# Low tail products of two up-projection steps set among attention scores, two attention chunks begun a step later

## The reference

```python
# 1: gated linear attention (mLSTM) per head, written as a recurrence over t
C = f_stab * C + i_stab * outer(v_t, k_t);  n = f_stab * n + i_stab * k_t
y_t = sigmoid(o_t) * (C @ q_t) / max(|n . q_t|, 1)
# 2: a dense layer pair, 320 -> 2048 -> 320
h = x @ w_in;  x = (h - tanh(h)) @ w_out
# 3: four experts, 320 -> 1024 -> 320, mixed by given probabilities
out += p[:, e] * (relu(x @ w1[e]) @ w2[e])
```

## Time and profile before

| | us |
|---|---|
| median of 3 runs | 585.32 |
| lowest, highest | 584.59, 585.38 |
| the profiled execution | 584.94 |
| its span, first to last instruction | 583.1 |
| TensorE matmuls busy | 579.0 |
| VectorE, ScalarE, GpSimd busy | 222.2, 200.9, 128.5 |

### The profile page before, as it was taken

How to read it: one execution, slowest core, us unless ns; L and a number is a source line. 1 busy time by engine, 2 the same in 40 slices (tenths; PEclk the granted TensorE clock), 3 DMA queues, 4 the chain that set the end, 5 groups by cost and what they waited for, 6 DMA issues and landing times.

```text
span 583.1 us, 8971 instructions
## 1 busy us (share of the span) xinstructions
PE 579.0 (99%) x3658; PEld 528.1 (91%) x3658; DVE 222.2 (38%) x449; ACT 200.9 (34%) x399; POOL 128.5 (22%) x102
## 2 busy tenths in 40 slices
PE   9999999999999999999999999999999999999997
PEld 8899999999998888899999999999999999999997
DVE  6657656565555333413131313131323232222222
ACT  5785655565444555511123211123211111111111
POOL 4888333332200444400004300014300000000000
PEclk9999999999999999999999999999999999999999
DMA  7987735664210222300002300001000000001011
GB/s 277 349 289 254 273 106 169 168 168 97 52 40 0 75 96 98 127 5 1 0 1 99 100 1 0 1 1 49 2 1 1 1 0 1 1 0 46 1 45 46
DMA packets 39054, 44.33 MB, mean 76 GB/s; under 512 B 21190, under 2 KB 31686, under 8 KB 39014
## 3 DMA queue, kind: packets, MB, share of 16 engines
q1 hardware_dynamic: 38912, 43.71, 23.3%
q10 hardware_dynamic: 102, 0.05, 0.0%
HBM read 39.02 MB, written 4.73 MB: 75 GB/s over the span
## 4 chain that ended last, share of the span: by engine, by line
PE 99%; DVE 0%; issue 0%; ACT 0%; DVEq 0%
PE bank L1321 11%; PE bank L1320 11%; PE bank L1322 11%; PE bank L1376 10%; PE bank L1375 10%; PE bank L1374 10%; PE bank L1323 6%; PE bank L1324 6%; PE bank L1346 5%; PE bank L1347 4%; PE bank L1348 4%; PE bank L1118 2%; PE bank L1354 2%; PE bank L1355 2%; PE bank L1161 1%; PE bank L1132 1%
## 5 line engine op out<-in xcount | busy, mean ns | idle before, releaser
L1094 DVE SCALAR_TENSOR_TENSOR g_lo<-bank,g_hi 128x512 fp32r<-128x512 f32 x96 | 66.4, 692 | 253.4 <-ACT g_hi L815 253.4
L815 ACT ACTIVATE g_hi<-bank 128x512 fp32r<-128x512 f32 x96 | 57.5, 599 | 269.8 <-PE bank L1324 269.7
L1376 PE MATMUL bank<-w_all,g_lo 128*128 128x320 f32 x384 | 118.7, 309 | 0.0
L1375 PE MATMUL bank<-w_all,g_hi 128*128 128x320 f32 x384 | 118.5, 309 | 0.0
L1321 PE MATMUL bank<-x_lo,w_all 128*128 128x512 f32 (+2 forms) x318 | 118.2, 372 | 0.0
L1374 PE MATMUL bank<-w_all,g_hi 128*128 128x320 f32 x384 | 118.2, 308 | 0.0
L1320 PE MATMUL bank<-x_hi,w_all 128*128 128x512 f32 (+2 forms) x318 | 117.9, 371 | 0.0
L1322 PE MATMUL bank<-x_hi,w_all 128*128 128x512 f32 (+2 forms) x318 | 117.0, 368 | 0.0
L598 POOL TENSOR_TENSOR w_all<-w_raw,w_all 128x1408 fp32r<-128x1408 f32 x16 | 51.7, 3233 | 192.3 <-ACT w_all L687 192.3
L1374 PEld LDWEIGHTS bank<-w_all,g_hi 128*128 128x128 f32 x384 | 72.1, 188 | 3.7
L1375 PEld LDWEIGHTS bank<-w_all,g_hi 128*128 128x128 f32 x384 | 72.1, 188 | 3.7
(11 more groups left out here) (161 smaller groups left out, 646.0 us busy)
## 6 DMA issues: line engine op xcount, KB each, us to landing
w_raw<-in_w SPq DMA_DIRECT2D x24, 704.0 KB, 4.3
zb<-z SPq DMA_DIRECT2D x10, 512.0 KB, 5.3
feat<-in_feat SPq DMA_DIRECT2D x10, 512.0 KB, 4.1
tok<-in_tok SPq DMA_DIRECT2D x10, 484.0 KB, 4.8
spare<-xg SPq DMA_DIRECT2D x8, 256.0 KB, 2.8
out<-arena SPq DMA_DIRECT2D x12, 160.0 KB, 1.9
fb<-f SPq DMA_DIRECT2D x16, 80.0 KB
xg<-feat SPq DMA_DIRECT2D x16, 80.0 KB
```

What stands on the lines that cost most here:

```text
L815: A(g_hi[:, b, 0:N], h_ps[b][:, 0:N], ACT.Relu).then_inc(ghi_ready, 1)
L1094: V.scalar_tensor_tensor(g_lo[:, b, 0:N], h_ps[b][:, 0:N], 0.0, g_hi[:, b, 0:N].bitcast(F32), ALU.max, ALU.subtract).then_inc(g_ready, 1)
L1375: mm(out, g_hi[:, b, t], low_w, start=False, stop=False)
L1376: last = mm(out, g_lo[:, b, t], high_w, start=False, stop=stop)
```

## The change

Each of chunks 6 to 11 names a step `m = START[n] + 1`, the step of its scores: with the new `START`, 19, 23, 27, 32, 36 and 39. In `up(m)` and in `up(m+1)` the matmul L1324 is left out. In its place the scores hold two pairs of half-size matmuls, `halves`: each has 64 rows and half of the 384 columns, one in the lower and one in the upper 64 partitions, and one writes to the bank of step m, the other to that of step m+1. The first pair comes after two of the eight score matmuls and begins the bank of step m+1 there; the second comes after six and ends that of step m, so that `h_ready` of step m is now given there. That the upper 64 rows can be used asks for the high tail there: for the second half of the columns of a group `x_low` now writes the low tail in the lower 64 partitions. The middle chunks 3 and 6 are written in two pieces for it. Chunks 9 and 10 begin a step later (31 and 35), so that steps m and m+1 always belong to one group.

```diff
-START = {2: 3, 3: 7, 4: 10, 5: 14, 6: 18, 7: 22, 8: 26, 9: 30, 10: 34, 11: 38}
+START = {2: 3, 3: 7, 4: 10, 5: 14, 6: 18, 7: 22, 8: 26, 9: 31, 10: 35, 11: 38}
...
+def tail_parts(n):
+    if n in (3, 6):
+        return (True, slice(0, CH // 2)), (False, slice(CH // 2, CH))
+    return (n not in (4, 7), slice(0, CH)),
...
+        in_halves = [START[n] + 1 for n in range(6, STEPS)]
...
-                V.scalar_tensor_tensor(x_hi[64:P, 2, c], turn[64:P, 2, :], 0.5, x_hi[64:P, 2, c].bitcast(F32),
-                                       ALU.mult, ALU.subtract).then_inc(xlo_done, 1)
+                for above, t in tail_parts(n):
+                    half, ct = slice(64, P) if above else slice(0, TAIL), slice(n * CH + t.start, n * CH + t.stop)
+                    last = V.scalar_tensor_tensor(x_hi[half, 2, ct], turn[half, 2, t], 0.5,
+                                                  x_hi[half, 2, ct].bitcast(F32), ALU.mult, ALU.subtract)
+                last.then_inc(xlo_done, 1)
...
+            def halves(m, here, there):
+                N = width(m)
+                c, half = span(m).start, N // 2
+                mm(h_ps[here % 2][:, 0:half], up_part(here, 1, 2)[0:TAIL, :], x_hi[0:TAIL, 2, c:c + half],
+                   start=False, stop=False)
+                return mm(h_ps[there % 2][:, half:N], up_part(there, 1, 2)[64:P, :], x_hi[64:P, 2, c + half:c + N],
+                          start=there != m, stop=there == m)
...
                 r = n % RING
+                m = START[n] + 1 if n >= BATCH else -1
...
+                    if j == 0 and m in in_halves:
+                        pe.wait_ge(g_ready, m)
+                        halves(m, m, m + 1).then_inc(halves_begun, 1)
+                    if j == 2 and m in in_halves:
+                        pe.wait_ge(halves_begun, in_halves.index(m) + 1)
+                        halves(m, m + 1, m).then_inc(h_ready, 1)
                 last.then_inc(s_ready, 1)
...
+                begun = m - 1 in in_halves
                 for k in range(2 if m else 0):
-                    mm(h, up_part(m, 0, k), x_hi[:, k, c], start=k == 0, stop=False)
+                    mm(h, up_part(m, 0, k), x_hi[:, k, c], start=k == 0 and not begun, stop=False)
...
-                mm(h, up_part(m, 0, 2), x_hi[:, 2, c], start=False, stop=False)
-                mm(h, up_part(m, 1, 2), x_hi[:, 2, c], start=False, stop=True).then_inc(h_ready, 1)
+                last = mm(h, up_part(m, 0, 2), x_hi[:, 2, c], start=False, stop=begun)
+                if begun:
+                    last.then_inc(h_ready, 1)
+                elif m not in in_halves:
+                    mm(h, up_part(m, 1, 2), x_hi[:, 2, c], start=False, stop=True).then_inc(h_ready, 1)
```

More of the change, by code:

```diff
@@ L272, in mlstm_mlp_experts @@
         part_lo = sem("part_lo")
+        halves_begun = sem("halves_begun")
         xhi_done = sem("xhi_done")
```

## The result

| | before | after |
|---|---|---|
| median, us | 585.21 | 589.13 |
| lowest, highest (6 executions each) | 584.49, 585.38 | 586.89, 591.13 |
| the profiled execution, its span | 584.94, 583.1 | 586.89, 585.0 |
| TensorE matmuls busy, by the page | 579.0 | 577.9 |

The ratio after to before is 1.0071, interval 1.0053 to 1.0088: 0.7% slower, where 586.7 us (+0.3%) was forecast with a range up to 588.0. The direction is right, and the profiled execution, 586.89, lies on the forecast. But it is the fastest of the six; the median lies 2.4 us above the forecast and outside its range. So two questions are open: whether the sum held in the execution that was profiled, and what the other executions have that it has not.

A forecast was written before the change was run, and what follows sets the result against it. TensorE's matmuls, busy 99% of the span, were taken as the bound. Terms -0.81 + 0.15 - 0.12 + 0.03 + 0.34 + 2.2 = +1.8 on 584.94 gave 586.7 us; range for 8 in 10: 584.9 to 588.0.

The forecast's parts named there:

- What bounds the kernel: Whole kernel: TensorE's matmuls are busy 579.0 us, 99% of the span, so only removed matmuls or new standstills change the time.
- The pairs: Among the scores, six times: two pairs at 0.107 us each replace two matmuls at 0.174; net -0.81 us.
- that rival (0.02): Around the scores: 64 and 40 rows are two tiling modes and TensorE drains between them, +3.6 us, 590.3; chance 0.02.
- the one with dear pairs: Among the scores: pairs don't run side by side or wait for their weights, 0.174 or more each, 587.7 us; chance 0.06.
- The self-wait: In the scores: the second pair waits for the first, with 0.1 us to spare; nothing, at most 0.1 each.
- `h_ready(m)` late: After the scores: h_ready comes some 0.9 us later, delaying tanh, subtraction and g_lo, but TensorE has other work; nothing.
- `down(32)`: Between down(31) and down(32): the sums of chunk 9, moved there, cover the wait for the evacuation; -0.12 us.
- (a) `state_ready`: Step 39, before the scores of chunk 11: they wait for finish_state(10), now at the end of step 38's VectorE work; +0.34 us.
- (b) the denominators: DMA queue, steps 39 to 43: chunk 11's denominators are read at 161.98, land at 164.3 and delay down(43); +2.2 us.
- the wait at step 31: Scores at step 31: the first pair waits for g_ready, late because of step 30's VectorE work; +0.15 us.
- two plain steps: Steps 30 and 34 now end with x_low and no scores behind; weights come slightly late, +0.03 us net.
- the DMA chain is slower: DMA queue before down(43): other transfers lengthen a leg by 1 us and the stall equally, 587.7 us; chance 0.15.

The follow-up runs named there:

- the repeat: The changed kernel measured once more, unchanged, against the kernel before: 589.63 us, ratio 1.0092.

## Why the prediction was right, and where it failed

- **What bounds the kernel** held: each us of standstill on TensorE came out as a us of time.
- **The pairs** were sized nearly rightly: 0.11 us each against 0.107, and 0.174 for what they replace. Net -0.6 against -0.81 over six places. The Trainium skill (TensorEngine Tiling, Key Properties) has the engine drain between tiling modes; the rows from 120.67 to 121.99 leave no room for that between 40 and 64 rows (two pairs cost 0.22 in all), so that rival (0.02) is out, as is the one with dear pairs.
- **The self-wait** on `halves_begun` cost nothing, **`h_ready(m)` late** cost nothing, **`down(32)`** gave its 0.12, each as reckoned.
- **(a) `state_ready`** came out at +0.33 against +0.34.
- **(b) the denominators** came out at 161.94 and 164.33 against 161.98 and 164.3, and the hole at 2.1 against 2.2; moving them in the queue took the stall away. The main mechanism was found. That its price agrees to 0.1 us is luck in part: the working left out a lead of 0.9 us and the 0.8 by which GpSimd lengthened L994 and L977.
- **Missed inside (b)**: "VectorE is late there, but `down(39)` is far." The working had the second scores operation over at 153.08. I held it against `down(39)` only, and not against the sums, which need those scores and stand before `down(39)`. By the working's own numbers they would have asked for them at 153.16 (L1161 at 153.29, 0.35 less for two L1324, 0.22 more for two pairs), so it would have shown 0.1 us to spare and no wait. What made the 0.34 is the duration that it took for x_low(9): 0.44, where L994 took 0.82. By luck the -0.3 at the start of the kernel and the wait at step 31 that didn't show in this execution made up for it (in the repeat step 31 has +0.26).
- **The step that failed** is the last: "584.94 + 1.8 = 586.7". The sum prices one execution with every other duration left as it was, and takes it for the median, which measured 589.13. Two mechanisms were not in it at all, neither in a term nor in a rival.

First, **the clock**. The hole was priced at its own length. In the two executions that were traced with a mean clock of 0.997 it is followed by 3.4 us at half the granted clock, which cost 1.6 us in each. Over the 18 executions of the changed kernel, its repeat and the new START alone: 10 have this mean clock and a median of 590.3 us, 7 have 0.999 or more and a median of 588.0; one has 0.994. Filled with idle matmuls or shortened to 0.40 us, the hole has no such sequel in 21 of 22 executions. That the mean clock of the untraced ones comes from the same place is inferred from this.

Second, **GpSimd beside VectorE**. I took x_low at 0.44 and 0.32 at the places to which START moved it, from one step where GpSimd was idle. At steps 30 and 34 GpSimd's cut of z and weighing of v, set off by a DMA whose landing varies, fall beside it or not. Where they do, its two operations took up to 1.24 and 0.82 (step 30 of the kernel with chunk 9 alone a step later). At step 39 GpSimd's scaling of q, set off by the scores, falls beside x_low(9) in all five profiles of kernels with the changed START, the pairs and x_low(9) in that step: 0.81 or 0.82 each time. The forecast's "+0.03" for two plain steps had looked at TensorE and VectorE alone, and took steps with 0.36 and 0.26 us to spare for as safe as one with 1.32. At steps 30, 31 and 34 this cost 0.37 us in the trace of the repeat, 1.1 in that of START alone (0.36 at step 30, 0.77 at step 34) and nothing in the first profile. At step 39 it cost 0.34 us in the first profile too, and by the estimate above some 0.5 of the hole. Even the executions at full clock have a median of 588.0, 1.3 above the forecast; the traces point to this mechanism, but how much of the 1.3 it carries in executions without a trace isn't settled.

My range failed with the step: its upper end came from a slower DMA queue, and it held nothing for what a standstill does afterwards, or for durations that vary with a neighbour engine. The rival "the DMA chain is slower" gave 587.7, near the executions at full clock but for a reason that no trace shows.

Left open: six executions with a mean clock of 0.994, three of kernels with the change or parts of it (589.46 to 593.25 us) and three of the kernel before (588.65 to 590.22), which has no such stall. None of them has a trace; 0.994 over 590 us would be about 7 us at half clock, two stretches like the traced one (an estimate). Open too is why kernels without the hole at step 43 show 0.996 or 0.997: six executions of eleven with chunk 9 alone a step later, four of the ten in which GpSimd waits for x_low, one each of two others. Nor did I find out why the same hole is followed by the fall of the clock in some executions and not in others: the two profiles of the changed kernel differ there by 0.1 us in the length of the hole.

## What to carry to other kernels

A hole in a TensorE-bound stream costs more than its length, and not each time: price it with and without a stretch at half clock behind it, and let the range hold both. When an operation of VectorE moves to another step, look at what GpSimd does there and how far its start depends on a DMA, and compare the delay with the smallest slack of the new step; one profile shows only one such coincidence. And when a working gives a late time, hold it against every consumer of that result, not only the next big one, and write down the smallest slack: at the sums it was 0.1 us, and one lengthened operation went through it.

## What the runs showed of the hardware

- VectorE operations with two inputs in SBUF are blocked by GpSimd's. x_low's first operation took 0.40 to 0.43 us in all 75 cases without GpSimd beside it, all eight of the kernel before among them, and in six with an overlap of under 0.2 us; in the other 23, with GpSimd's operation begun first, it took 0.44 to 1.24 and was over 0.28 us after GpSimd's, each time (0.275 to 0.286). So it doesn't share, it waits. The gate took 0.49 without and 1.05 to 1.58 with it, an operation on 128 by 8 elements 0.17 and up to 0.76. Operations that read a PSUM bank (g_lo, L876) kept their 0.56 and 0.68. Where VectorE's operation began first, GpSimd's grew: weighing v from 0.74 to 0.90, scaling q beside the gate from 1.30 to 1.54. The Trainium skill (SBUF — State Buffer, Who interferes with whom) says that the two engines share one port pair, held by one of them for a whole instruction, and that a VectorE instruction with two SBUF inputs contends with a GpSimd instruction that reads SBUF. By that rule, the traces agree in which operations are hit; it is the rule that should have been weighed for steps 30, 34 and 39.
- After a standstill of 2.4 us and then 1.4 us of renewed work (the repeat) or 0.35 us (START alone), TensorE's granted clock was 0.50 for 3.4 us, then full again; the changed kernel with a standstill of 2.3 us also ran on at 1.00.
- A pair of 64-row matmuls of 192 columns among 40-row ones cost 0.11 us, no more than a pair of 40-row ones of 128 columns (0.11), with no price to be seen for the change of height.
